# Attention scores and weight transposes in two row halves of the array, each half with its own PSUM bank

## The reference

```python
# q, k, v: (4 batches, 8 heads, 576 rows, 64)
scores = scale * q @ k.T                          # per batch and head, 576 x 576
x = log1p(|i - j|) / log1p(max(i, 1))             # positions i, j
scores += (relu(x * w1 + b1) @ w2)[head]          # 32 hidden units, 8 heads
attn = exp(scores - max(scores)); attn /= sum(attn) + 1e-9
x = (attn @ v), heads side by side                # 2304 tokens x 512
noisy = x @ w_gate + log1p(exp(x @ w_noise)) * noise
out[token] = sum over its top 2 experts e: weight * relu(x @ w1[e]) @ w2[e]
```

## Time and profile before

| what | value |
|---|---|
| time, median of 3 runs | 881.62 us (879.67 to 883.56) |
| the profiled execution | 881.9 us, span 880.0 us |
| TensorE products, busy | 815.1 us, 93% |
| VectorE, busy | 520.8 us, 59% |
| ScalarE, busy | 414.0 us, 47% |
| GpSimd, busy | 365.9 us, 42% |

### The profile page before, as it was taken

One profiled execution on the slowest core, in us unless ns is written; L12 is line 12 of the kernel. 1 busy time (PEld: TensorE's weight loads), 2 busy tenths in 40 slices (PEclk: granted clock), 3 DMA queues, 4 the chain that ended last, 5 costly groups with the idle time before them and its releaser, 6 DMA issues.

```text
span 880.0 us, 17622 instructions
## 1 busy us (share of the span) xinstructions
PE 815.1 (93%) x5598; PEld 668.2 (76%) x5598; DVE 520.8 (59%) x1172; ACT 414.0 (47%) x856; POOL 365.9 (42%) x376
## 2 busy tenths in 40 slices
PE   4868999999999999619999999999999999999995
PEld 1327777777777777318989889899898898998983
DVE  6967888888888888595343533624435336344311
ACT  5986777777777777512322322423223233232200
POOL 2006676676667677133144232432442324322312
PEclk9998999999999999958999999999999999999998
DMA  8784333443253441617047163380461633803113
GB/s 177 215 224 133 110 99 109 121 128 112 85 170 90 116 144 54 246 39 276 2 75 237 29 157 127 60 232 19 81 230 36 148 127 60 250 3 48 14 22 39
DMA packets 51471, 102.15 MB, mean 116 GB/s; under 512 B 12704, under 2 KB 17440, under 8 KB 51424
## 3 DMA queue, kind: packets, MB, share of 16 engines
q1 hardware_dynamic: 40240, 79.85, 29.4%
q0 software_dynamic: 10320, 21.41, 13.3%
q10 hardware_dynamic: 864, 0.29, 0.2%
HBM read 70.38 MB, written 20.53 MB: 103 GB/s over the span
## 4 chain that ended last, share of the span: by engine, by line
PE 84%; DMA 5%; DVE 4%; ACT 3%; issue 2%; POOL 0%; SPq 0%; POOLq 0%; DVEq 0%; ACTq 0%
PE ps L757 26%; PE po L772 23%; PE pt L557 12%; PE ps L551 10%; PE po L622 10%; DMA slab<-work 2%; DMA out_rows<-ys,iscat 2%; ACT work L1122 2%; ACT work L1115 1%; PE po L557 1%; DVE ohlo L1008 1%; DMA w2blk<-in_w2b 1%; DVE wlo L859 1%; PE ps L534 0%; PE po L604 0%
## 5 line engine op out<-in xcount | busy, mean ns | idle before, releaser
L757 PE MATMUL ps<-xT,whi 128*128 128x320 f32 x1024 | 177.2, 310 | 0.9 <-ACT xT L1240 0.9
L1251 ACT ACTIVATE hT<-ps 128x320 fp32r<-128x320 f32 x128 | 56.0, 437 | 233.2 <-PE ps L757 213.2
L772 PE MATMUL po<-whi,hT 128*128 128x512 f32 x640 | 162.5, 398 | 0.0
L757 PEld LDWEIGHTS ps<-xT,whi 128*128 128x128 f32 x1024 | 157.2, 189 | 1.7 <-issue 1.1
L1055 DVE SCALAR_TENSOR_TENSOR hT<-ps,hT 128x320 fp32r<-128x320 f32 x128 | 62.9, 492 | 154.4 <-ACT hT L1251 134.7
L1309 POOL TENSOR_SCALAR work<-work,rcp 128x576 f32<-128x576 f32 (+1 forms) x160 | 117.5, 744 | 85.2 <-DVE rcp L855 84.8
L840 DVE CUSTOM_DVE_ANT_0 ns<-ps,slab 128x576 f32<-128x576 f32 (+1 forms) x160 | 120.3, 752 | 33.1 <-PE ps L551 26.2
L772 PEld LDWEIGHTS po<-whi,hT 128*128 128x128 f32 x640 | 118.1, 188 | 26.9
L1150 ACT ACTIVATE work<-ns,nmax 128x576 f32<-128x576 f32 (+1 forms) x160 | 123.7, 773 | 26.3 <-DVE nmax L840 26.2
L1343 POOL DMA_INDIRECT out_rows<-ys,iscat x40 | 68.2, 1704 | 135.4 <-DMA out_rows<-ys,iscat 72.2
L557 PE MATMUL pt<-cst,work 128*128 128x128 f32 (+3 forms) x800 | 113.7, 269 | 2.4 <-DVE work L871 1.1
(11 more groups left out here) (131 smaller groups left out, 1012.8 us busy)
## 6 DMA issues: line engine op xcount, KB each, us to landing
wraw<-in_mw SPq DMA_DIRECT2D x64, 512.0 KB, 11.2
slab<-work SPq DMA_DIRECT2D x36, 288.0 KB, 3.8
qraw<-in_qT SPq DMA_DIRECT2D x66, 144.0 KB, 2.8
kraw<-in_kT SPq DMA_DIRECT2D x66, 144.0 KB, 2.9
vs<-in_v SPq DMA_DIRECT2D x32, 160.0 KB, 4.0
out_rows<-zeros SPq DMA_DIRECT2D x32, 152.0 KB
x_rows<-xnat SPq DMA_DIRECT2D x8, 576.0 KB, 5.2
wrow<-w_rows,iscat POOLq DMA_INDIRECT x40
```

What stands on the lines that cost most here:

```text
L757: mm = nc.tensor.matmul(bank, w1s[i][pw][:, c, f * P:(f + 1) * P], xT[px][:, c, half * HB:(half + 1) * HB], start=j == 0 and c == 0, stop= ...
L772: mm = nc.tensor.matmul(po[:, (i + t) % 2, :], hT[px][:, c, t * P:(t + 1) * P], w2s[i][pw][:, c, :], start=j == 0 and c == 0, stop=j == 2 ...
L1251: nc.scalar.activation(hT[0][:, f, half * HB:(half + 1) * HB], ps[n % 4 // 2][:, n % 2, 0:HB], ACT.Relu)\
```

## The change

The head's two 64-row halves of the array are used as two arrays. For the scores, q's high and low parts stand in tiles of their own (`qh`, `ql`), each with the same 64 values in both partition halves; k's first 288 columns stand in partitions 0 to 63 and the last 288 in 64 to 127 (`kh`, `kl`, 288 wide in place of 576). A tile's scores are three products per half, half 0 into one bank of `ps` and half 1 into the other, the two halves in turn. The missing fourth combination, low times low, is left out; before, the stationary operand with both parts of q brought it in.

For the transposes, rows 0 to 63 of a tile go to `pt[0]` and rows 64 to 127 to `pt[1]`, five transposes of 64 rows x 128 columns each, in turn. The rows of `E` are 640 wide, with 64 columns that GpSimd clears once, so that the fifth column tile is like the others and granules 4 and 5 fall away. A full tile fills both banks, tile 4 only bank 1. VectorE copies bank 0 of tiles 0 to 3 (320 columns), ScalarE bank 1 of all five tiles. In `ptr` a wait and a semaphore step stand for each bank, ahead of all transposes of the tile.

```diff
-def ptiles(t):
-    u = (t - LAG) % NU
-    return [u] if u < NU - 1 else [4, 5]
+def banks(u):
+    return (0, 1) if u < NU - 1 else (1,)
...
-                for half in range(2):
-                    for i, kk in enumerate((kh, kl)):
-                        mm = nc.tensor.matmul(ps[sl][:, half, 0:HALF], qs[h % 2][:, u * P:(u + 1) * P],
-                                              kk[h % 2][:, half * HALF:(half + 1) * HALF],
-                                              start=i == 0, stop=i == 1)
+                for i, (qq, kk) in enumerate(((qh, kh), (ql, kh), (qh, kl))):
+                    for half in range(2):
+                        part = slice(half * D, (half + 1) * D)
+                        mm = nc.tensor.matmul(ps[sl][:, half, 0:HALF], qq[h % 2][part, u * P:(u + 1) * P],
+                                              kk[h % 2][part, :], start=i == 0, stop=i == 2)
...
-            def ptr(now, kind, b, h, k):
+            def ptr(now, kind, b, h, u):
...
+                e = E[(h % 2) * NU + u]
+                pe.wait_ge(norm_done, n * NU + u + 1)
+                for bank in banks(u):
+                    pe.wait_ge(t_done[bank], C_T + granule(bank, ("p", h, u), now, kind))
                     pe.sem_inc(pe_passed, 1)
...
+                last = {}
+                for kt in range(NU):
+                    for half in range(2 if u < NU - 1 else 1):
+                        part = slice(half * D, (half + 1) * D)
+                        bank = half if u < NU - 1 else 1
+                        last[bank] = nc.tensor.transpose(pt[bank][:, kt * D:(kt + 1) * D], e[part, kt * P:(kt + 1) * P],
+                                                         ident[part, part])
+                for bank, mm in last.items():
+                    mm.then_inc(t_ready[bank], 1)
...
+                nc.vector.tensor_copy(PT[h % 2][:, :, k * P:k * P + D],
+                                      pt[0][:, 0:NU * D].rearrange("p (k s) -> p k s", k=NU)).then_inc(t_done[0], 1)
...
-                        if u % 2 == 0:
+                        if u < NU - 1:
                             evac0(b, kind, x[0], h, u)
...
+                at = k * P + (D if k < NU - 1 else 0)
+                nc.scalar.activation(PT[h % 2][:, :, at:at + D], pt[1][:, 0:NU * D].rearrange("p (k s) -> p k s", k=NU),
+                                     ACT.Copy).then_inc(t_done[1], 1)
...
-                        if u in (1, 3, 4):
-                            evac1(b, kind, x[0], h, 5 if u == 4 else u)
+                        evac1(b, kind, x[0], h, u)
...
             act.preload_act_table_set("natural_log_exp_and_others")
+            evac1(B, "drain", -1, H - 1, 0)
             evac1(B, "drain", -1, H - 1, 1)
             softplus(range(CL), 0)
-            evac1(B, "drain", -1, H - 1, 3)
-            evac1(B, "drain", -1, H - 1, NU)
+            for u in range(2, NU):
+                evac1(B, "drain", -1, H - 1, u)
...
-                nc.gpsimd.tensor_scalar(qhi[:, :].bitcast(F32R), qraw[h % 2][:, :], low[:, 0:1], 1.0, ALU.mult, ALU.mult)\
+                nc.gpsimd.tensor_scalar(qh[h % 2][:, 0:S], qraw[h % 2][:, :], 1.0, 1.0, ALU.mult, ALU.mult)\
...
-            for i in range(2):
-                nc.gpsimd.memset(PT[i][LAST:P, NU - 1, :], 0.0).then_inc(pt_zeroed, 1)
-                pool.wait_ge(pt_zeroed, i + 1)
+            nc.gpsimd.memset(epads, 0.0).then_inc(pt_zeroed, 1)
```

More of the change, by code:

```diff
@@ L112, in granules @@
 def granules(t):
-    return [(k % 2, ("p", (t - LAG) % SLOTS // NU, k), t < LAG) for k in ptiles(t)]
+    h, u = divmod((t - LAG) % SLOTS, NU)
+    return [(bank, ("p", h, u), t < LAG) for bank in banks(u)]
 ORDER = [[(e, before) for t in range(SLOTS) for bank, e, before in granules(t) if bank == i] for i in range(2)]
@@ L131, in issued @@
 def issued(bank, h, k, now, kind, batch):
-    body = batch + (h * NU + min(k, NU - 1) + LAG >= SLOTS)
+    body = batch + (h * NU + k + LAG >= SLOTS)
     if body == 0:
@@ L206, in build @@
         wnoise = tmp("wnoise", [P, NT, NE])
-        work = tmp("work", [P, 2 * NU * S * 2])
+        work = tmp("work", [P, 2 * NU * (NU * P + S)])
         slab = tmp("slab", [P, NU * H * S])
         bias = slab[:, :].rearrange("p (u h s) -> p u h s", u=NU, h=H)
-        E = [work[:, i * S:(i + 1) * S] for i in range(2 * NU)]
-        PT = [work[:, (2 + i) * NU * S:(3 + i) * NU * S].rearrange("p (k s) -> p k s", k=NU) for i in range(2)]
+        EW = NU * P
+        E = [work[:, i * EW:(i + 1) * EW] for i in range(2 * NU)]
+        epads = work[:, 0:2 * NU * EW].rearrange("p (i w) -> p i w", i=2 * NU)[:, :, S:EW]
+        PT = [work[:, 2 * NU * EW + i * NU * S:2 * NU * EW + (i + 1) * NU * S].rearrange("p (k s) -> p k s", k=NU)
+              for i in range(2)]
         hid = [[work[:, (i * GS + k) * S:(i * GS + k + 1) * S] for k in range(GS)] for i in range(NHID)]
@@ L220, in build @@
         qraw = [tmp(f"qraw{i}", [P, S]) for i in range(2)]
[L221 to L224, removed]
+        kraw = [tmp(f"kraw{i}", [P, HALF]) for i in range(2)]
+        qh = [tmp(f"qh{i}", [P, NU * P], F32R) for i in range(2)]
+        ql = [tmp(f"ql{i}", [P, NU * P], F32R) for i in range(2)]
+        kh = [tmp(f"kh{i}", [P, HALF], F32R) for i in range(2)]
+        kl = [tmp(f"kl{i}", [P, HALF], F32R) for i in range(2)]
         vs = [tmp(f"vs{i}", [P, NU, D]) for i in range(4)]
@@ L610, in pv @@
                 if kt == 0:
-                    for bank, k in ((0, 4), (1, 5)):
+                    for bank, k in ((0, NU - 2), (1, NU - 1)):
                         pe.wait_ge(t_done[bank], C_T + issued(bank, h, k, now, kind, batch))
@@ L636, in batch @@
                         h, u = divmod(x[1], NU)
-                        for k in ([u] if u < NU - 1 else [4, 5]):
-                            ptr(b, kind, b + x[0], h, k)
+                        ptr(b, kind, b + x[0], h, u)
                     if burst:
@@ L671, in tile_of @@
             def tile_of(u):
-                for k in ([u] if u < NU - 1 else [4, 5]):
-                    ptr(B, "drain", B - 1, H - 1, k)
+                ptr(B, "drain", B - 1, H - 1, u)
             tile_of(0)
@@ L1147, in expo @@
                     if h >= 2 or kind == "loop":
-                        for bank, k in ((0, 4), (1, 5)):
+                        for bank, k in ((0, NU - 2), (1, NU - 1)):
                             act.wait_ge(t_ready[bank], issued(bank, (h - 2) % H, k, now, kind, batch - (h < 2)))
-                nc.scalar.activation(E[i][0:r, :], ns[t % 2][0:r, :], ACT.Exp, bias=nmax[0:r, i:i + 1], scale=-1.0,
+                nc.scalar.activation(E[i][0:r, 0:S], ns[t % 2][0:r, :], ACT.Exp, bias=nmax[0:r, i:i + 1], scale=-1.0,
                                      accum_out=ssum[0:r, i:i + 1]).then_inc(exp_done, 1)
```

57 lines of the change are left out of this document (12 added, 45 removed).

## The result

| | before | after |
|---|---|---|
| time, median (same chip) | 882.59 us | 907.73 us (903.23, 904.11, 911.35, 914.81) |
| ratio, 95% interval | | 1.0292 [1.0206, 1.0378] |
| profiled execution, span | 880.0 us | 913.0 us |
| first to last score reduction (attention) | 280.9 us | 307.1 us |
| the four batches in it | 67.2, 72.1, 72.1, 69.4 | 69.6, 79.5, 82.3, 75.7 |

The forecast was 885 us, between 865 and 903. Slower, the outcome with the highest chance, was right; the time is 23 us off and outside the range. The profiled execution of after is the longest of its four, so its parts add up to 33 us, not 25: start +1.8, attention +26.2, drain +3.8, routing and experts +1.2.

What follows compares the result with a forecast made beforehand. TensorE bounded the kernel before; after, a closed loop of waits: head 9.05 against 8.96, times 31, +2.8, start -0.6, drain +1.5, first batch -0.6. 881.9 + 3.1 = 885 us, range 865 to 903.

Steps and rivals of the forecast that it cites:

- Row halves side by side: Attention on TensorE: both halves run together, scores 0.41 us a tile for 0.54, ten transposes 0.33 for 0.44.
- Rivals B and C: Attention: B, weight loads of row halves don't overlap, 931, chance 0.11; C, halves' products run one after another, 941, chance 0.05.
- The loop of waits: Attention, per head: closed loop through TensorE and VectorE, each piece waiting for the last: 8.88 us, TensorE idle some 2.
- double wait: From a copy's end to the next transposes, TensorE waits for both copies: 0.25 us, twice a head.
- rival A: Attention: shorter loop, second wait and shape change cost nothing, reduction starts 0.06 sooner; head 8.47, 868 us, chance 0.17.
- extras: Attention: token transposes and gate products that don't hide in idle time, 0.17 us a head for 0.46 before.
- rival D: Attention: TensorE's clock could fall with idle time; a half-clock head about 6 us more, two give 897; chance 0.07.
- Start: Before attention's products: one clear of 10 x 64 columns replaces two of 576 columns, TensorE waits for them: -0.6 us.
- Drain: Last head: transposing tile 1 waits for ScalarE's tile 0 copy behind a table load: +1.5 us, between 0 and 2.

Runs made afterwards that it cites:

- two_unrolled: The changed kernel without the third score product (q's high part times k's low part), TensorE's batches written out instead of looped: 880.84 us, ratio to before 0.9979.
- transposes_only: The changed kernel with the scores of the kernel before, so only the transposes use row halves: 917.53 us, ratio to before 1.0416.
- short_copies: after_unrolled with both copies of a tile's transposes cut from 320 to 64 columns: 877.84 us, one execution.
- after_unrolled: The changed kernel with TensorE's batches 1 to 3 written out in place of the loop: 889.89 us, ratio to before 1.0109.
- early_scores: after_unrolled with the scores of the next head's tile 0 issued ahead of the transposes of tile 4: 892.21 us, ratio to before 1.0116.
- scores_only: The kernel before with the changed scores alone (three products in row halves), transposes as before: 893.19 us, ratio to before 1.0137.

## Why the prediction was right or wrong

- **Row halves side by side (right).** The two products of a score pair start 3 ns apart, or some 30 ns right behind transposes, and pairs follow each other every 0.13 us; of the transposes one starts every 0.031 us. Scores take 0.45 a tile including the first step, 0.41 forecast; ten transposes 0.31 to 0.33, 0.33 forecast. Rivals B and C fell. A weight load of 64 rows and 128 columns for a transpose lasts 0.14 us, longer than the 0.107 that the prediction cites from the Trainium skill, and ten of them start 0.031 us apart, so several are under way at once. That the halves run at once agrees with what I cited from the Trainium skill's page "TensorE: Matmul & The Clock Gate", section "Part 3: Packing small matmuls", and not with the reading that loads queue up behind each other.
- **The loop of waits (right in its form; the number is in part luck).** Three edits changed a piece and moved the plain head by as many pieces as the loop has: three score tiles (two_unrolled, transposes_only) and two copies (short_copies). 8.88 forecast, 8.76 in the first batch of after_unrolled. Copy 0.49 measured; hand-over with the double wait 0.25 (in after_unrolled VectorE's copy starts at 210.54, ends 0.49 later, transposes at 211.29), so rival A, in which the second wait costs nothing, fell too. But other pieces were off and cancelled. In the head from 104.12 to 112.88 us transposes and the scores behind them take 0.98 twice, not 0.79; copy 2 starts as the transposes end, not 0.20 later; from value products to reduction 0 it is 1.13, not 1.31, and from there to copy 0 0.96, not 1.10. TensorE is idle for 1.29 us of this head, 0.79 ahead of transposes 1 and 0.33 ahead of transposes 3, where I had some 2. The mean head with all extras, 9.05 in after_unrolled and 9.05 forecast, agrees because the extras cost more than my 0.17 by what the loop cost less. It holds only without the loop in TensorE's program, and early_scores showed that this loop has a second way beside it, of nearly the same length.
- **The loop in the program (missed).** This is the step that failed. My sum took the loop of waits as the whole cost of a head, 31 times 9.05 us, and put the jumps back of TensorE's loop and the thresholds of its waits at nothing without a reason: I counted what each instruction costs and not how many there are. By the profiles it is 9.3 + 7.0 us at the two jumps, with the half clock that follows, and 0.14 to 0.4 for each other looped head, some 4 us. With the batches written out the same kernel takes 889.9 us, 5 above the forecast and within the range. The profile before had the sign of it: queue 8 falling silent from 204 us, at the end of the second batch. The Trainium skill's page "Runtime: NRT & Kernel Launch", section "Instruction fetch mechanics", has the mechanism: a taken branch to code outside the fetched window waits for a fetch, and TensorE's store holds 2048 instructions. The traces agree with a limit of that order, though by it 1,861 should still fit; where the section speaks of a window of two pages they don't agree, since bodies of some seven loads of 16 KB were kept. The price, 3.2 + 1.5 us a jump without a product, is only in the traces.
- **The clock (named as rival D, its chance too small, its price per head too large; part of the result).** At the start of attention, where TensorE waits for VectorE, the granted clock is at its lower level, 1.2 GHz, for 24 us (PEclk 0.51 from 66 to 90 us), where before it was two stretches of 7 and 3.4 us; in after_unrolled, with the same long stretch, the head that ends in it takes 10.73 (9.13 before), where the plain heads behind it take 8.76, +2.0. The stretch from 141.6 to 145 us cost 1.8. I had put a head at half clock at 6 us more, as if TensorE's own work bounded it. I had also priced the clock as a case of its own, D at 0.07; it came as the aftermath of idle stretches, at the start, behind the jumps and in the drain.
- **Start (right in size, hidden).** The clear takes 0.63 where two took 1.20. It began 2.6 us later in the profile of after because the bias table, which the change doesn't touch, came later; in after_unrolled it began at 65.64, as before (65.22).
- **Drain (mis-sized).** +1.5 forecast; counted from the last reduction, the last value product comes 3.8 us later in after, 6.2 in after_unrolled. The mechanism was the one named:

```profile
354.55 1.28 ACT L1201 ACT_TABLE_LOAD   x1
355.85 0.44 ACT L1151 ACTIVATE work<-pt 128x320 f32<-128x320 f32 x1
...
356.43 0.53 PE L571 MATMUL pt<-cst,work 64*128 64x64 f32 x10 [1.98 <-ACT work L1151]
```

The wait is 1.98, and in after_unrolled half clock follows it from 357.6 to 371.2 us. Moving the copy took 3.0 us out (17.9 to 14.9).

Two slips of arithmetic in the prediction change nothing: ten transposes one by one at 0.06 us are 0.60, not 0.62, which takes 2 us off rivals B and C; and the chances of the cases add up to faster 0.25, same 0.27, slower 0.48, not 0.24, 0.30 and 0.46.

What stays open: why the clock falls in one idle stretch and not in another.

## What to carry to other kernels

Before an edit that multiplies the instructions inside a loop on one engine, count the loop body and look in the profile at whether its instruction queue is silent once the body has run once; if it would no longer be, price each jump at several us and its aftermath in the clock, or write the loop out. A profile shows such a jump as a long branch record on that engine. Work on an array that is cheaper per tile gains nothing when its result buffers go from two in turn to one pair filled at once: write the closed loop through both engines down first, with every way through it, since shortening one leaves the other. And halves of the array must be used by neighbours alike: a change of shape between them, 0.15 us, is larger than the 0.09 that the split saves on a tile of scores.

## What the runs showed of the hardware

- A jump back to a body of 1,861 records on TensorE holds the branch for 3.8 us (3.2 without a product) and then stops TensorE for 1.5 us more; each stall ends 1.3 to 1.4 us after a load of 16 KB on queue 8. With bodies of 1,294 to 1,701 records the branch takes 0.2 us and nothing is loaded again. Written out, the same code streams in unnoticed.
- Waits with thresholds from a register cost TensorE more than waits with constants, 0.25 us per head with some 18 arithmetic operations, where the waits are in the critical loop; where TensorE has work queued (the kernel before) nothing of it is seen.
- Semaphore steps on TensorE are not free: 16 per step, 1,920 in all, made the kernel 174 us longer, at most 0.09 each (the jumps are in it).
- Each change of the shape in which TensorE's array is used costs 0.15 us (0.59 for 0.44): between 64 and 128 rows for scores and transposes (scores_only), and from the column strips of value products to full width (before).
